# Batch 0's attention: order of loads, one normalising instruction a step, weight casts in later steps, the last pair's low part on VectorE

## What is computed

```
scores = where(mask, q @ k.T / 8, -1e9); attn = exp(scores - max) / sum        # heads 0-3: 32 last positions
x  = attn @ v, heads side by side                                            # heads 4-7: same position mod 32
h  = gelu_tanh(x @ w_in); u, v = halves of h;  v_n = layernorm(v) * g_ln
x  = x + (u * (w_sg @ v_n + b_sg)) @ w_out                                   # stage A
x  = x + relu(layernorm(x) * g2 @ w_ch1) @ w_ch2                             # stage B
```

## Time and profile before

| | before |
|---|---|
| median of 3 executions | 688.06 us (687.66 to 690.57) |
| profiled execution, its own time | 690.06 us |
| its span | 688.2 us |
| PE, PEld busy | 663.7, 627.1 us |
| DVE, ACT, POOL busy | 548.8, 354.0, 253.5 us |
| DMA | 98.26 MB, 143 GB/s mean |
| chain that ended last | PE 64%, issue 15%, DVE 8%, POOL 7%, DMA 3%, ACT 2% |

### The profile page before, as it was taken

The page is one execution under the profiler, slowest core; times in us unless marked ns, Lnnn a source line. Parts: engine busy times, 40 slices in busy tenths (PEclk is TensorE's granted clock), DMA queues, the critical chain, the costliest instruction groups (busy, mean ns, idle before and its releaser), DMA issues.

```text
span 688.2 us, 14199 instructions
## 1 busy us (share of the span) xinstructions
PE 663.7 (96%) x5158; PEld 627.1 (91%) x5160; DVE 548.8 (80%) x1305; ACT 354.0 (51%) x894; POOL 253.5 (37%) x261
## 2 busy tenths in 40 slices
PE   7799999999999999899999999999989999999997
PEld 4569888999889988899999999999989999999997
DVE  5867995899679966997876785697989599796993
ACT  5765683488347854244554363345574354344440
POOL 0459331624252346558435356333001414112121
PEclk9999999999999999899999999999999999999999
DMA  8651005200440015108443667869851724526301
GB/s 287 249 176 59 2 1 200 104 1 2 135 187 1 2 36 191 55 24 285 146 155 109 198 231 250 305 193 344 294 174 34 288 91 172 209 70 247 133 18 51
DMA packets 49012, 98.26 MB, mean 143 GB/s; under 512 B 4656, under 2 KB 32176, under 8 KB 46256
## 3 DMA queue, kind: packets, MB, share of 16 engines
q1 hardware_dynamic: 48240, 96.16, 40.1%
q0 software_dynamic: 704, 1.21, 0.7%
HBM read 64.83 MB, written 32.52 MB: 141 GB/s over the span
## 4 chain that ended last, share of the span: by engine, by line
PE 64%; issue 15%; DVE 8%; POOL 7%; DMA 3%; ACT 2%; SPq 1%; DVEq 0%; POOLq 0%; ACTq 0%
PE pair L1840 11%; PE pair L1842 11%; PE pair L1841 11%; PE pair L1631 7%; PE pair L1633 7%; PE pair L1632 7%; PE pair L1688 3%; PE pair L1670 3%; PE pair L1655 2%; DVE stage L1504 2%; POOL xr L986 1%; POOL vn_lo L839 1%; DMA w_raw<-w_ff_dram 1%; POOL res L538 1%; POOL rstd_v L834 1%
## 5 line engine op out<-in xcount | busy, mean ns | idle before, releaser
L1840 PE MATMUL pair<-xf_hi,w_hi 128*128 128x288 f32 x896 | 266.9, 298 | 5.4 <-DVE w_lo L518 2.7
L1841 PE MATMUL pair<-xf_lo,w_hi 128*128 128x288 f32 x896 | 265.3, 296 | 0.0
L1842 PE MATMUL pair<-xf_hi,w_lo 128*128 128x288 f32 x896 | 264.4, 295 | 0.0
L1840 PEld LDWEIGHTS pair<-xf_hi,w_hi 128*128 128x128 f32 x896 | 168.7, 188 | 7.6 <-issue 4.2
L1842 PEld LDWEIGHTS pair<-xf_hi,w_lo 128*128 128x128 f32 x896 | 169.4, 189 | 0.0
L1841 PEld LDWEIGHTS pair<-xf_lo,w_hi 128*128 128x128 f32 x896 | 168.9, 188 | 0.0
L1100 ACT ACTIVATE xf_hi<-res 128x576 fp32r<-128x576 f32 x140 | 93.2, 681 | 98.5 <-PE pair L1842 55.2
L1504 DVE TENSOR_TENSOR stage<-pair,stage 128x576 f32<-128x576 f32 x136 | 100.8, 753 | 43.0 <-PE pair L1842 37.4
L565 DVE TENSOR_TENSOR xf_lo<-res,xf_hi 128x576 fp32r<-128x576 f32 x140 | 109.3, 799 | 3.4 <-ACT xf_hi L1100 3.4
L986 POOL TENSOR_TENSOR xr<-xr,stage 128x576 f32<-128x576 f32 x16 | 36.3, 2266 | 163.5 <-DVE stage L1504 163.3
L1188 ACT ACTIVATE stage<-stage 128x576 f32<-128x576 f32 x64 | 43.5, 683 | 88.5 <-DVE stage L1504 88.4
(11 more groups left out here) (133 smaller groups left out, 1297.6 us busy)
## 6 DMA issues: line engine op xcount, KB each, us to landing
hid_scratch<-stage SPq DMA_DIRECT2D x64, 288.0 KB, 3.2
res<-hid_scratch SPq DMA_DIRECT2D x16, 1152.0 KB, 6.5
w_raw<-w_ff_dram SPq DMA_DIRECT2D x16, 512.0 KB, 4.2
v_sb<-vW_dram SPq DMA_DIRECT2D x16, 384.0 KB, 7.1
x_scratch<-res SPq DMA_DIRECT2D x4, 1152.0 KB, 5.3
xr<-x_scratch SPq DMA_DIRECT2D x16, 288.0 KB, 2.9
out_dram<-xr SPq DMA_DIRECT2D x16, 288.0 KB, 2.3
k_sb<-kT_dram SPq DMA_DIRECT2D x15, 304.0 KB, 7.0
```

Source lines behind the costliest of these rows:

```text
L1840: pe.matmul(dst, wh, xh, start=(start and x == 0), stop=False)
L1841: pe.matmul(dst, wh, xl, start=False, stop=False)
L1842: last = pe.matmul(dst, wl, xh, start=False, stop=(stop and x == n - 1))
```

## The change

Seven edits, most of them in the first attention alone:

1. Loads: v of pair 0 and the mask of heads 4-7 are issued behind q and k of pair 1, and no longer ahead of them.
2. `normalise`: the four `tensor_scalar` of a twin become one `tensor_tensor` over all four tiles, with the reciprocals as an operand that is repeated along the row. This one holds for all 48 twins.
3. `SOLO_SPLIT`: the DVE casts of w_in stand in steps 5, 7, 8, 10 (v half) and 11, 12, 13, 14 (u half). None is left behind the loop. POOL's order follows.
4. The mask's cast for heads 4-7 goes from DVE to POOL, at its start.
5. The low part of the last pair (`xop_lo` 3) goes from POOL to DVE, right behind its rounding, in every batch.
6. ACT: the table of the gelu is loaded ahead of batch 0's first gelu, and the five casts of w_sg go behind the fourth and fifth gelu and the first of the u half.
7. DVE: the low parts of w_sg follow two tokens' steps later.

```diff
-SOLO_SPLIT = {4: (0,), 5: (1,), 6: (2,), 7: (3,)}
+SOLO_SPLIT = {5: (0,), 7: (1,), 8: (2,), 10: (3,), 11: (4,), 12: (5,), 13: (6,), 14: (7,)}
...
                     if first and pair == 0:
                         sp.dma_start(eye_f[:], eye).then_inc(eye_in, 16)
-                    blocks = slice(2 * PER_PAIR * pair, 2 * PER_PAIR * (pair + 1))
-                    sp.dma_start(v_sb[:, blocks, :], vW[b, :, blocks, :]).then_inc(v_in[pair], 16)
-                    if first and pair == 0:
+                        continue
+                    for i in range(2) if first and pair == 1 else (pair,):
+                        blocks = slice(2 * PER_PAIR * i, 2 * PER_PAIR * (i + 1))
+                        sp.dma_start(v_sb[:, blocks, :], vW[b, :, blocks, :]).then_inc(v_in[i], 16)
+                    if first and pair == 1:
                         sp.dma_start(mask_raw[:, 2 * P:3 * P], masks[:, 2 * P:3 * P]).then_inc(class_mask_in, 16)
...
+            pool.wait_ge(class_mask_in, 16)
+            pool.tensor_copy(mask_b[:, 2, :], mask_raw[:, 2 * P:3 * P]).then_inc(class_ready, 1)
...
-                if first:
-                    for s in range(NS):
-                        split_wsg(s)
                 for s in range(NS):
                     gelu_v(b, s)
+                    if first and s >= NS - 2:
+                        split_wsg(2 * s - 2 * NS + 4)
+                        split_wsg(2 * s - 2 * NS + 5)
...
-                for j in range(2):
-                    for h in range(2):
-                        e = probs_at(s, j, h)
-                        last = dve.tensor_scalar(e, e, stat_at(row_inv, s, j, h), None, ALU.mult)
-                last.then_inc(probs_ready, 1)
+                nk = BLOCKS[2 * s][2]
+                e = probs[0:nq, s % 4, 0:4 * nk].rearrange("p (g k) -> p g k", g=4)
+                inv = row_inv[0:nq, 4 * s:4 * s + 4].unsqueeze(2).broadcast_to([nq, 4, nk])
+                dve.tensor_tensor(e, e, inv, ALU.mult).then_inc(probs_ready, 1)
...
+            def split_x(b, pair):
+                dve.wait_ge(x_hi, b * PAIRS + (pair + 1))
+                dve.wait_ge(x_lo, b * PAIRS + pair)
+                dve.tensor_tensor(xop_lo[:, pair, :], res_at(b, pair, 0, S), xop_hi[:, pair, :].bitcast(F32),
+                                  ALU.subtract).then_inc(x_lo, 1)
...
             round_x(0, PAIRS - 1, quad=False)
-            for c in range(KC):
-                split_win(1, c)
+            split_x(0, PAIRS - 1)
```

More of the change, by code:

```diff
@@ L297, in sequence_block_kernel @@
         wsg_in, wout_in = sem("wsg_in"), sem("wout_in")
-        const_ready = sem("const_ready")
+        const_ready, class_ready = sem("const_ready"), sem("class_ready")
         power_ready = sem("power_ready")
@@ L914, in period @@
                         split_gated(b, 2 * t)
-                    if t in QUAD_X:
+                    if t in QUAD_X and QUAD_X[t] < PAIRS - 1:
                         split_x(b + 1, QUAD_X[t])
@@ L934, in last_period @@
                     sum_weights(g)
+            pool.wait_ge(class_mask_in, 16)
+            pool.tensor_copy(mask_b[:, 2, :], mask_raw[:, 2 * P:3 * P]).then_inc(class_ready, 1)
             split_win(0, 0)
+            split_x(0, 0)
             split_win(0, 1)
-            split_x(0, 0)
             split_win(0, 2)
+            split_x(0, 1)
             split_win(0, 3)
-            split_x(0, 1)
+            split_win(1, 0)
             split_x(0, 2)
-            split_x(0, 3)
-            for c in range(KC):
+            for c in range(1, KC):
                 split_win(1, c)
@@ L1106, in gelus @@
                     act.wait_ge(b_const, 3)
+                act.wait_ge(power_ready, 1)
+                act.activation(table_c[:], minus_half[:], ACT.Gelu_apprx_tanh)
                 if norm:
-                    act.wait_ge(power_ready, 1)
-                    act.activation(table_c[:], minus_half[:], ACT.Gelu_apprx_tanh)
                     for h in range(2):
@@ L1117, in gelus @@
                         squares(n, h)
-                if first:
-                    for s in range(NS):
-                        split_wsg(s)
                 for s in range(NS):
                     gelu_v(b, s)
+                    if first and s >= NS - 2:
+                        split_wsg(2 * s - 2 * NS + 4)
+                        split_wsg(2 * s - 2 * NS + 5)
                 for g in range(NS, NGELU):
                     gelu_u(b, g)
+                    if first and g == NS:
+                        split_wsg(NS - 1)
                     if first and g - NS >= GC:
@@ L1260, in _ @@
             dve.wait_ge(const_ready, 1)
[L1262 to L1265, removed]
             def split_win(half, c):
@@ L1375, in norm_all_v @@
                         v_norm(b, s - 1)
-                    if first and s < NS:
-                        split_wsg(s)
+                    if first and s >= 2:
+                        split_wsg(s - 2)
                     if b in (1, 2) and s in (1, 2, 3):
@@ L1418, in period @@
                         round_x(b + 1, QUAD_X[t])
+                        if QUAD_X[t] == PAIRS - 1:
+                            split_x(b + 1, PAIRS - 1)
                     if t < QUADS:
@@ L1474, in _ @@
                 if s == 2 * PER_PAIR:
-                    class_mask()
+                    dve.wait_ge(class_ready, 1)
                 if s < TWINS:
```

## The result

| | before | after |
|---|---|---|
| median | 687.86 us (687.39 to 690.57) | 679.14 us (677.40 to 680.29) |
| ratio | | 0.9864 [0.9844, 0.9883] |
| profiled execution, its span | 690.06, 688.2 us | 680.29, 678.5 us |
| mean granted clock of it | 0.989 | 0.995 |

What follows compares the result with a forecast made beforehand. PE bounds the kernel, in the loop through a ring with DVE. Gains 2.8 + 1.6 less 1.7 for a clock fall make 2.7: 690.06 becomes 687.4, or 685.8 from the median with 0.4 taken off; range 682.4 to 688.8.

Steps and rivals of the forecast that it cites:

- The start: From the first attention's loop to the u half: gain 2.8 us, less 1.7 for a clock fall in a new 2.4 hole.
- the rivals without a hole or without a fall: Behind the loop: no hole, 681.6 us, chance 0.08; or a hole where the clock holds, 684.1 us, chance 0.27.
- Loads, 0.95: Loop, step 3: pair 1's k lands near 9.2, not 10.55, so scores start at 9.84, not 10.79; gain 0.95 us.
- the 9.8 to 9.9 that I gave as a sign: Loop: scores of step 3 were to start at 9.8 to 9.9, with clock 1.00 through 14.
- Clock, 1.1: Loop: with 0.28 us of the k hole left, the clock fall at 10.86 goes too; gain 1.1, bounds 0 and 1.1.
- 0.8 and part of the 1.2: Loop: 0.8 us from faster `normalise` in four steps; 1.2 from multiplications blocked once, not twice, and smaller blocks.
- The first woven attention: Transposes trailing the multiplications by 0.10 to 0.15 us at seven of twelve places no longer do; gain 1.6 us.
- The rate: `normalise`: one multiplication takes 0.67 us for 512 columns, 0.56 for 432, 0.47 for 360, against 0.87 for the old four.
- rival 3: Loop and later woven attentions: the one multiplication runs at half rate, 1.2 us for 512 columns; 694 us, chance 0.08.
- In the second and third woven attention transposes come 0.3 to 1.9 us behind the multiplications: nothing to gain: Later woven attentions: transposes do not closely follow the multiplications, so faster `normalise` was given no gain.
- The last pair's subtraction on DVE delays two additions there by half a microsecond ...: nothing: Second and third woven attentions: PE wants the delayed additions' banks 1.4 us later, so the subtraction's move changes nothing.
- Rival 4: Before stage B: POOL's weight sums wait for a load, not PE, so the start's gain is lost; 687.6 us, chance 0.12.

Runs made afterwards that it cites:

- e11: Kernel before with only the new order of loads (v of pair 0 and mask behind pair 1's q and k): 689.29 us, ratio 1.0006.
- e1: Kernel before run again with no edit: 688.80 us, ratio 1.0006.
- e9: Kernel before with the one multiplication for four in batch 0's attention (the loop) alone: 683.57 us, ratio 0.9932.
- e10: Kernel before with the one multiplication for four in the three woven attentions alone: 686.37 us, ratio 0.9961.
- e5: Changed kernel with the last pair's low part put back on POOL in the three woven attentions: 683.49 us, ratio 0.9929.
- e13: Kernel before with POOL's rstd load in the last period put behind its first two weight sums: 687.63 us, ratio 0.998.
- e6: Kernel before with the one multiplication, and the last pair's low part on DVE in the three woven attentions: 679.26 us, ratio 0.9864.
- e7: Changed kernel with eight products of zeros put on PE into the hole behind the loop, before chunk 3: 679.88 us, ratio 0.9878.
- e8: Kernel before with 64 semaphore increments added to PE's instructions at its start, shifting its code: 694.88 us, ratio 1.0102.

## Why the prediction was wrong

**The start** came near what was laid out. Loop end 37.65 (37.3), PE on at 42.57 (42.5), clock 0.50 behind it for 3.4 us, cost 1.7 (1.7). Gain 1.24 where 2.8 - 1.7 = 1.1 was written, and the rivals without a hole or without a fall did not come. That this sum fits is in part luck. "Loads, 0.95" measured 0.1 (e11): in the second trace of the same kernel (e1) the scores of step 3 start at the same time without that wait. In the changed kernel the scores of step 3 start at 10.31, not at the 9.8 to 9.9 that I gave as a sign. "Clock, 1.1" took the fall to hang on that wait; in e1 and e11 the wait is gone and the fall has moved to 24.4. What took it out of the loop is the multiplication, which brings 4.3 by itself (e9), the clock among it, where I gave it 0.8 and part of the 1.2. And the subtraction ended at 42.43 (42.4), behind a hole of 1.95 and not of 2.4.

**The first woven attention**: 2.2 for 1.6, the place right and the term 0.6 too small. PE's holes go altogether (0.85 of idle time), and the transposes that trailed follow at once.

**The rate** of the one multiplication: 0.69 for 96 x 512 (0.67 written), 0.61 for 432 columns, 0.53 for 360, against 0.87 for the old four; rival 3 is refuted. The Trainium skill ("VectorE: DVE Perf Modes", The perf-mode tier table) would, by that table alone, have had it the other way; the rows decide.

**The step that failed first** is "In the second and third woven attention transposes come 0.3 to 1.9 us behind the multiplications: nothing to gain". It asked only whether PE waits for DVE. The two stops of 0.79 and 0.72, whose rows say "issue", stood in the trace that I read, and I took what has no releaser as something that no edit can touch. They are PE waiting for its code, and they go with the four multiplications: 2.0 us (e10 without them, e9 with them).

**The second** is "The last pair's subtraction on DVE delays two additions there by half a microsecond ...: nothing". I priced the instruction where it arrives, and not what stood behind it where it left: POOL's issue of the rstd load, which moved 2.6 us up against PE and out of the way of w_raw (e5, e13). That is 1.4 us in the hole, and with it the 6.8 us stretch of low clock, 2.6 more.

Rival 4 named the very place (POOL's weight sums before stage B, which wait for a load) and had its sign wrong: that load is issued on PE's progress, so it held nothing back, and the change made it faster.

What stays open: how much of the low clock one may count on. e6 and e7 each won 1 to 1.5 us by the trace that their medians don't show, and e11, whose clock did not fall behind its hole of 3.02 us, was 2.6 ahead of the kernel before at 291 and 0.1 at the end.

## What to carry to other kernels

When an instruction leaves an engine, read what was queued behind it there, DMA issues above all, and which transfer those then meet. Treat a stop marked "issue" in a busy PE as a cost that an edit elsewhere can remove, and look at PE's code loads beside it. Before you price a wait, see whether a second execution of the same kernel has it. And measure each part alone before adding parts: here one instruction alone brought as much as all seven edits, and the six others, 6.1 us alone, added nothing to it.

## What the runs showed of the hardware

- PE can run out of code in mid-stream: 0.3 to 1.1 us a time at eleven of 34 places, where the load began 2.2 to 2.8 us ahead. The Trainium skill ("Runtime: NRT & Kernel Launch", Instruction fetch mechanics) calls the cost of such a boundary "mostly hidden"; here 41 loads of 16 KB agree with its block size, and two of them were not hidden in the kernel before.
- 64 semaphore increments ahead of PE's first product made it 9.3 us later, some 0.15 each (e8: at 10.56, not 1.30).
- A load of 512 KB took 6.3 us from its issue to the first sum with a spread load of 288 KB issued 3.7 us ahead of it, and 6.8 to 7.7 with it 1.2 ahead.
- The clock after a hole, one execution each: after holes of 1.60 to 1.68 us before the mix it held in all six traces; after 1.83 to 3.02 it fell in nine of eleven (it held in e8, 2.93, and e11, 3.02). The hole of 1.92 to 1.95 behind the loop was followed by a fall in all five traces that have it. But around the hole of 1.65 to 1.67 in the old loop it fell in four of six (e1, e8, e11, e13), and in the other two (before, e10) it fell elsewhere in the loop. So a hole's length alone does not tell.
